# Products behind the last one that nothing reads: eight distances in memory between moving tile and weights, in two forms

## The chip, the cores and the metric

The kernel runs on one core of one Trainium2 chip. The metric is the device time of one execution in microseconds (us); of the kernel before there are two timed executions, with a median of 1193.43 us (1192.92 and 1193.94).

## The reference

Three layers are computed over 8192 tokens of 192 channels in float32: a causal mixing over seven tokens with softmaxed taps per head, a gated network, and a second network with the ELU function.

```
w   = softmax(weight)                      # 8 heads x 7 taps
x   = sum over k of w[h, k] * x[s + k - 6] # causal, per head of 24 channels
y   = (silu(x @ w_gate) * (x @ w_val)) @ w_out1      # 192 -> 1536 -> 192
out = elu(y @ w_in2) @ w_out2                        # 192 -> 2048 -> 192
```

## The kernel before, in words

Tokens are taken in 16 chunks of T = 512. Each chunk goes through a mix phase (12 steps, the gated network) and an ELU phase (8 steps j, each with two blocks of 128 hidden units). A float32 operand is kept as two float32r parts, hi and lo, and a product of two operands is made as three products: hi by hi, lo weights by hi, hi weights by lo. 192 channels are 128 and 64, so most products have 64 rows of contraction. They are issued in pairs, one on partitions 0 to 63 (TOP) and one on partitions 64 to 127 (LOW), into two banks of PSUM; `both` (L921) and `third` (L888) issue such pairs and `mm` (L885, its products are recorded at L886) issues every product.

Two forms of pair matter here. In the **up form** (`third`, also `both` in `down`), the weights are 128 columns of a weight tile and the moving tile is 512 columns of activations. In the **token form** (`by_tokens`, L948), the roles change: 128 columns of activations (`hid_hi` or `hid_lo`) are loaded as weights and the rows of `out2_w` move past them, 384 columns for the hi part and 192 for the lo part, hi and lo in turn.

The weights of the up form lie in `up1_w` and `up2_w`, their moving tiles in `in_a` and `in_b`, each with three slots of 512 columns (MAIN, CROSSED, TWICE). The sizes of all the tiles between `in_a_hi` and `hid_lo`, and of those between `up1_w_hi` and `out2_w`, are multiples of 128 columns (512 bytes), and so are the steps from one slot or weight block to the next.

Each engine runs its own instruction stream, with semaphores between them. In TensorE's stream the mix and ELU phases of chunks 2 to 14 stand in a hardware loop; what comes before and behind is written out. The last of it are `elu_phase(CHUNKS - 1)`, `elu_phase(CHUNKS)` and `last_blocks` (L977). `last_blocks` ends with products over all 128 rows into the four banks Z; each of the last four results is announced on `last_z`. Then ScalarE copies half of each bank to `result` (L660), VectorE adds the other half (L726), and SyncE and ScalarE store two blocks each (L332). SyncE at last waits until all stores have landed (L418). At the end of the program all engines meet.

At the beginning TensorE makes products on zeros and on the identity (`warm`, L1074), whose results nothing reads.

Of the kernel before, what the change touches and what calls it, by code (L numbers as in the profile page):

```python
# [28 lines left out]
P = 128  # L29


def mix_ffn_ffn(nc, x, weight, w_gate, w_val, w_out1, w_in2, w_out2, out):
    BATCH, SEQ, D = x.shape
# [4 lines left out]
    T = 512  # L38
# [34 lines left out]
    with ctx:  # L73
        def sb(name, shape, dt=F32):
            return ctx.enter_context(nc.sbuf_tensor(name, shape, dt))
# [5 lines left out]
        up1_w = {part: sb(f"up1_w_{part}", [P, PARTS, F1], F32R) for part in ("hi", "lo")}  # L81
# [5 lines left out]
        out2_w = sb("out2_w", [P, N2, 2 * D], F32R)  # L87
# [24 lines left out]
        in_a = {k: sb(f"in_a_{k}", [P, PARTS, T], F32R) for k in ("hi", "lo")}  # L112
        in_b = {k: sb(f"in_b_{k}", [P, PARTS, T], F32R) for k in ("hi", "lo")}
        MAIN, CROSSED, TWICE = range(PARTS)
# [17 lines left out]
        up = [ctx.enter_context(nc.psum_tensor(f"up{i}", [P, T], F32)) for i in range(4)]  # L132
# [3 lines left out]
        TOP, LOW = slice(0, TAIL), slice(TAIL, P)  # L136
# [747 lines left out]
        def _(pe):  # L884
            def mm(dst, lhsT, rhs, start, stop):  # L885
                return nc.tensor.matmul(dst, lhsT, rhs, start=start, stop=stop, skip_group_check=True)  # L886
# [69 lines left out]
            def down2_pair(m, k0):  # L956
                two = (k0, k0 + 1)
                turns = 2 * (N2 // 2 * m + k0 // 2)
                if k0 == 0 and is_int(m, CHUNKS - 1):
                    pe.wait_ge(result_done, summed(m))  # L960
                elif k0 == 0:
                    pe.wait_ge(y_a, 2 * (m + 2))
                    pe.wait_ge(y_b, 2 * (m + 2))
                order = ((0, 2), (1, 3), (2, 0), (3, 1))
                for turn, (b, b_low) in enumerate(order if k0 // 2 % 2 == 0 else order[::-1]):
                    if turn >= 2:
                        pe.wait_ge(z_turn, turns + turn - 1)
                    for k in two:
                        pe.wait_ge(hi2_done, N2 * m + k + 1)
                        by_tokens(k, hid_hi, b, b_low, first=k == 0)  # L970
                        pe.wait_ge(lo2_done, N2 * m + k + 1)
                        end = by_tokens(k, hid_lo, b, b_low, last=k == N2 - 1)
                    if turn < 2:
                        end.then_inc(z_turn, 1)
                end.then_inc(down2_done, 2)

            def last_blocks():  # L977
                two = (N2 - 2, N2 - 1)

                def whole(b, k, data, last=False):  # L980
                    pe.wait_ge(hi2_done, N2 * (CHUNKS - 1) + k + 1)
                    if data is hid_lo and k == N2 - 1:
                        pe.wait_ge(last_lo_done, 1)
                    elif data is hid_lo:
                        pe.wait_ge(lo2_done, N2 * (CHUNKS - 1) + k + 1)
                    w = out2_w[:, k, 0:2 * D] if data is hid_hi else out2_w[:, k, 0:D]
                    cols = slice(0, 2 * D) if data is hid_hi else slice(0, D)
                    return mm(Z[b][:, cols], data[:, k % RING, b * P:b * P + P], w, False, last)

                down2_pair(CHUNKS - 1, N2 - 4)  # L990
                for b in (0, 1):
                    whole(b, N2 - 2, hid_hi)
                    whole(b, N2 - 2, hid_lo)
                    whole(b, N2 - 1, hid_hi)
                for b in (0, 1):
                    whole(b, N2 - 1, hid_lo, True).then_inc(last_z, 1)
                for b in (2, 3):
                    for k in two:
                        whole(b, k, hid_hi)
                        last = whole(b, k, hid_lo, k == N2 - 1)  # L1000
                    last.then_inc(last_z, 1)

            def input_ready(slot, n, hi, lo, crossed):
                if slot == CROSSED:
                    pe.wait_ge(crossed, 64 * (n + 1))
                else:
                    pe.wait_ge(hi, 2 * n + 1 + (slot == TWICE))
                    pe.wait_ge(lo, 2 * n + 1 + (slot == TWICE))

            def mix_phase(n):  # L1010
# [3 lines left out]
                for f in range(2 if chunk0 else 0, N1):  # L1014
                    if chunk0 and f in UP1_AT:
                        wait_weights(pe, UP1_AT[f])

                    if chunk0 and f >= 3:
                        pe.wait_ge(mul_done, f - 1)
                    elif chunk1 or f >= 2 and not chunk0:  # L1020
                        pe.wait_ge(mul_done, N1 * n + f - 1)
                    elif not chunk0:
                        pe.wait_ge(elu_done, N2 * (n - 2) + N2 - 2 + 2 * f)
                    ready = (lambda slot: input_ready(slot, n - 1, in1_hi, in1_lo, in1_crossed)) if f == 0 \
                        else lambda slot: None
                    gate, val = project(gate_bank(f, n), val_bank(f, n), up1_w, f, input1(n), ready)
                    gate.then_inc(gate_ready, 1)
                    val.then_inc(val_ready, 1)
                    if f < 2 and is_int(n, 2) and N2 - LAG2 + 2 * f in OUT2_AT:
                        wait_weights(pe, OUT2_AT[N2 - LAG2 + 2 * f])  # L1030
                    if f < 2 and not (chunk0 or chunk1):
                        down2_pair(n - 2, N2 - LAG2 + 2 * f)
                    if f == 0 and chunk1:
                        down1(0, N1 - 2)
                        down1(0, N1 - 1)
                    if f >= LAG:
                        if chunk0 and f - LAG in OUT1_AT:
                            wait_weights(pe, OUT1_AT[f - LAG])
                        if chunk0 and f == LAG:
                            pe.wait_ge(mul_done, LAG)  # L1040
                        down1(n, f - LAG)
                    if f == N1 - 1:
                        down1(n, N1 - LAG)

            def elu_phase(n):
                last = is_int(n, CHUNKS)

                for j in range(PAIR2):
                    if is_int(n, 1) and j in UP2_AT:
                        wait_weights(pe, UP2_AT[j])  # L1050

                    if j >= 2:
                        pe.wait_ge(elu_done, N2 * (n - 1) + 2 * j - 2)
                    elif last:
                        pe.wait_ge(elu_done, N2 * (n - 1) - 2 + 2 * j)
                    else:
                        pe.wait_ge(mul_done, N1 * (n + 1) - 1 + j)
                    ready = (lambda slot: input_ready(slot, n - 1, in2_hi, in2_lo, in2_crossed)) if j == 0 \
                        else lambda slot: None
                    even, odd = project(gate_bank(j), val_bank(j), up2_w, j, input2(n - 1), ready)  # L1060
                    even.then_inc(h2_ready, 1)
                    odd.then_inc(h2_ready, 1)
                    if j == 0 and last:
                        for k in range(N2 - LAG2, N2, 2):
                            down2_pair(n - 2, k)
                    elif j == 0:
                        down1(n, N1 - 2)
                        down1(n, N1 - 1)
                    if j >= 2:
                        if is_int(n, 1) and 2 * j - LAG2 in OUT2_AT:  # L1070
                            wait_weights(pe, OUT2_AT[2 * j - LAG2])
                        down2_pair(n - 1, 2 * j - LAG2)
# [39 lines left out]
            elu_phase(CHUNKS - 1)  # L1112
            elu_phase(CHUNKS)
            last_blocks()


# [16 lines left out]
```

## Time and profile before

| what | value |
|---|---|
| median of two executions | 1193.43 us |
| the profiled execution, its own time | 1192.35 us |
| its span, first to last instruction | 1190.5 us |
| TensorE products busy | 1184.2 us, 99% of the span |
| VectorE, GpSimd, ScalarE busy | 65%, 59%, 56% |
| granted TensorE clock, mean | 1.000 |

The profiled execution took 1.85 us more than its span; that is time outside the first and last instruction. Its own time is 1.08 us below the median. A busy time is the union of the recorded spans of an engine's instructions; ends of products are modelled, so how fast TensorE works is better read from the distance between starts.

### The profile page before, as it was taken

To read this page: it belongs to the slowest core of one execution; us is meant where nothing else is said; L and a number is where in the kernel's file an instruction comes from. 1 tells how busy PE (TensorE), PEld (TensorE's weight loads), DVE (VectorE), ACT (ScalarE), POOL (GpSimd) and SP (SyncE) were. 2 spreads that over 40 slices of the span, in tenths; PEclk is the share of its full clock that TensorE was granted. 3 is DMA by queue.
4 is the path that set the end of the run, shared out by engine and by line. 5 is a ranking of instruction groups with operands and counts; after the bars stand their busy time and mean duration, and the time that the engine had idled before them with its cause. 6 is when DMAs were issued, how large, how long until landed. Compare 5 with 4: busy or idle time off the path is not lost.

```text
span 1190.5 us, 31414 instructions
## 1 busy us (share of the span) xinstructions
PE 1184.2 (99%) x11804; PEld 1021.5 (86%) x11804; DVE 777.2 (65%) x1193; ACT 664.6 (56%) x1113; POOL 704.5 (59%) x520
## 2 busy tenths in 40 slices
PE   8999999999999999999999999999999999999999
PEld 7888889898888988889888898888988889888898
DVE  7887565685656766567665766657667475675675
ACT  6557555464554646546465564655646555465565
POOL 6389566474654746557465474654756556475565
PEclk9999999999999999999999999999999999999999
DMA  8422011121111211012110021100212002120110
GB/s 179 114 50 46 12 33 35 31 44 27 25 23 31 44 31 26 18 31 44 31 35 14 26 44 31 35 18 22 44 31 44 9 22 44 31 44 9 32 33 15
DMA packets 103956, 43.38 MB, mean 36 GB/s; under 512 B 75888, under 2 KB 93936, under 8 KB 103920
## 3 DMA queue, kind: packets, MB, share of 16 engines
q1 hardware_dynamic: 103104, 42.29, 16.5%
q10 hardware_dynamic: 816, 0.59, 0.2%
q8 instruction: 24, 0.39, 0.1%
q14 instruction: 12, 0.10, 0.0%
HBM read 16.12 MB, written 6.29 MB: 19 GB/s over the span
## 4 chain that ended last, share of the span: by engine, by line
PE 99%; DVE 1%; DMA 0%; ACT 0%; issue 0%; DVEq 0%; ACTq 0%
PE up L886 55%; PE down L886 43%; DMA taps_raw<-weight_dram 0%; DVE in_a_lo L854 0%; DVE in_a_lo L859 0%; PE down L1092 0%; ACT hidden L635 0%; DVE hidden L748 0%; DVE hid_lo L729 0%; ACT in_a_hi L640 0%; DVE in_b_lo L702 0%; DVE stage L726 0%; ACT stage L660 0%; ACT taps_exp L626 0%; DVE taps_head L834 0%
## 5 line engine op out<-in xcount | busy, mean ns | idle before, releaser
L444 POOL TENSOR_TENSOR hid_lo<-hidden,hid_hi 128x512 fp32r<-128x512 f32 x435 | 607.7, 1408 | 460.0 <-ACT hid_hi L583 299.4
L886 PE MATMUL down<-out_w,hid_hi 64*128 64x384 f32 x2040 | 300.0, 355 | 0.0
L748 DVE TENSOR_TENSOR hidden<-act,up 128x512 f32<-128x512 f32 x191 | 130.9, 686 | 238.4 <-ACT act L566 238.4
L886 PE MATMUL down<-out_w,hid_lo 64*128 64x192 f32 x2040 | 256.2, 247 | 0.0
L788 DVE TENSOR_SCALAR act<-up 128x512 f32<-128x512 f32 x256 | 164.9, 686 | 105.7 <-PE up L886 103.8
L886 PE MATMUL up<-in_b_hi,up_w_hi 64*128 64x512 f32 x1128 | 222.0, 390 | 0.0
L886 PE MATMUL up<-in_b_lo,up_w_hi 64*128 64x512 f32 x1128 | 221.3, 389 | 0.0
L886 PE MATMUL up<-in_b_hi,up_w_lo 64*128 64x512 f32 x1128 | 220.6, 388 | 0.0
L583 ACT ACTIVATE hid_hi<-hidden 128x512 fp32r<-128x512 f32 x192 | 121.6, 633 | 177.2 <-DVE hidden L748 160.2
L617 ACT ACTIVATE hid_hi<-hidden 128x512 fp32r<-128x512 f32 x256 | 157.0, 629 | 97.0 <-DVE hidden L804 80.2
L602 ACT ACTIVATE act<-act 128x512 f32<-128x512 f32 x256 | 156.1, 631 | 88.0 <-DVE act L788 88.0
L886 PEld LDWEIGHTS down<-out_w,hid_lo 64*128 64x128 f32 x2040 | 195.3, 187 | 5.3
L886 PEld LDWEIGHTS down<-out_w,hid_hi 64*128 64x128 f32 x2040 | 191.8, 184 | 5.4 <-issue 0.2
L566 ACT ACTIVATE act<-up 128x512 f32<-128x512 f32 x191 | 114.2, 598 | 146.0 <-PE up L886 144.7
L804 DVE SCALAR_TENSOR_TENSOR hidden<-act,up 128x512 f32<-128x512 f32 x256 | 168.8, 681 | 36.6 <-POOL hid_lo L444 29.3
L886 PE MATMUL down<-hid_hi,out_w 64*128 64x512 f32 x1152 | 163.1, 388 | 0.0
L886 PE MATMUL up<-in_a_hi,up_w_hi 64*128 64x512 f32 x786 | 155.8, 393 | 0.8 <-ACT in_a_hi L640 0.8
L886 PE MATMUL up<-in_a_lo,up_w_hi 64*128 64x512 f32 x786 | 155.1, 391 | 0.3 <-DVE in_a_lo L859 0.3
L886 PE MATMUL up<-in_a_hi,up_w_lo 64*128 64x512 f32 x786 | 153.4, 387 | 0.0
L696 DVE SCALAR_TENSOR_TENSOR mixed<-x_t,taps,mixed 128x512 f32<-128x512 f32 x192 | 141.7, 778 | 0.0
L886 PEld LDWEIGHTS down<-hid_hi,out_w 64*128 64x128 f32 x1152 | 108.1, 184 | 23.7
L886 PEld LDWEIGHTS up<-in_b_lo,up_w_hi 64*128 64x128 f32 x1128 | 105.8, 184 | 23.3
(98 smaller groups left out, 1082.6 us busy)
## 6 DMA issues: line engine op xcount, KB each, us to landing
x_raw<-x_dram SPq DMA_DIRECT2D x136, 64.0 KB, 2.2
out_dram<-stage SPq DMA_DIRECT2D x15, 384.0 KB, 2.7
in_b_hi<-in_b_hi SPq DMA_DIRECT2D x32, 128.0 KB, 2.3
in_b_lo<-in_b_lo SPq DMA_DIRECT2D x32, 128.0 KB, 2.3
swapped<-halves SPq DMA_DIRECT2D x32, 128.0 KB, 2.3
in_a_hi<-in_a_hi SPq DMA_DIRECT2D x30, 128.0 KB, 2.3
in_a_lo<-in_a_lo SPq DMA_DIRECT2D x30, 128.0 KB, 2.3
stage<-w_out_dram SPq DMA_DIRECT2D x7, 384.0 KB, 3.9
```

Of the source, the lines that this page charges most:

```text
L444: return pool.tensor_tensor(hid_lo[:, slot, :], hidden[:, s, :], hid_hi[:, slot, :].bitcast(F32), ALU.subtract)
L566: nc.scalar.activation(act[:, f % 2, :], gate_bank(f, n)[:, :], ACT.Silu)\
L583: nc.scalar.activation(hid_hi[:, f % RING, :], hidden[:, f % 2, :], ACT.Copy)\
L602: nc.scalar.activation(act[:, k % 2, :], act[:, k % 2, :], ACT.Exp).then_inc(exp_done, 1)
L617: nc.scalar.activation(hid_hi[:, k % RING, :], hidden[:, k % 2, :], ACT.Copy)\
L696: v.scalar_tensor_tensor(mixed[:, part, :], src, tap, mixed[:, part, :], ALU.mult, ALU.add).then_inc(mix_step, 1)
L748: v.tensor_tensor(hidden[:, f % 2, :], act[:, f % 2, :], val_bank(f, n)[:, :], ALU.mult)\
L788: v.tensor_scalar(act[:, k % 2, :], elu_bank(k)[:, :], 0.0, None, ALU.min)\
L804: v.scalar_tensor_tensor(hidden[:, k % 2, :], act[:, k % 2, :], -1.0, elu_bank(k)[:, :], ALU.add, ALU.max).then_inc(elu_done, 1)
L886: return nc.tensor.matmul(dst, lhsT, rhs, start=start, stop=stop, skip_group_check=True)
```

## The change

Behind `last_blocks()` in TensorE's stream a new function `spare_time()` is called. Nothing else is changed. It makes, without a wait and without a semaphore, 128 pairs in the up form and then 64 times two token-form pairs (hi and lo).

```diff
                         last = whole(b, k, hid_lo, k == N2 - 1)
                     last.then_inc(last_z, 1)
 
+            def spare_time():
+                line = 16
+                flat = {k: in_a[k][:, :, :].rearrange("p s t -> p (s t)") for k in ("hi", "lo")}
+                upper, lower = up[1], up[2]
+                for r in range(8):
+                    for i in range(16):
+                        both(upper, lower, up1_w["hi"][:, MAIN, i % 8 * P:(i % 8 + 1) * P],
+                             flat["hi"][:, r * line:r * line + T], True, True)
+                for r in range(8):
+                    for i in range(8):
+                        for part, cols in (("hi", 2 * D), ("lo", D)):
+                            held = flat[part][:, r * line:r * line + P]
+                            for bank, rows in ((upper, TOP), (lower, LOW)):
+                                mm(bank[:, 0:cols], held[rows], out2_w[rows, i, 0:cols], True, True)
+
...
             elu_phase(CHUNKS)
             last_blocks()
+            spare_time()
```

The moving tile of the up form and the held tile of the token form start r times 16 elements (64 bytes) into `in_a`, for r from 0 to 7. The banks `up[1]` and `up[2]` and the tile `in_a` are not used by any other instruction at that time.

## Rows read from the trace of the kernel before

**Rows 1.** The page: span, busy time and instructions of TensorE, granted clock in 40 slices.

```profile
span 1190.5 us, 31414 instructions
PE 1184.2 (99%) x11804; PEld 1021.5 (86%) x11804; DVE 777.2 (65%) x1193; ACT 664.6 (56%) x1113; POOL 704.5 (59%) x520
PEclk9999999999999999999999999999999999999999
```

**Rows 2.** The page: the chain that ended last, by engine.

```profile
PE 99%; DVE 1%; DMA 0%; ACT 0%; issue 0%; DVEq 0%; ACTq 0%
```

**Rows 3.** Timeline of the end: start us, length us, engine, line, operation, tiles.

```profile
1187.18 0.36 PE L886 MATMUL down<-out_w,hid_hi 128*128 128x384 f32 x1
...
1187.38 0.25 PE L886 MATMUL down<-out_w,hid_lo 128*128 128x192 f32 x1
1187.66 0.33 ACT L660 ACTIVATE stage<-down 128x192 f32<-128x192 f32 x1 [0.24 <-PE down L886]
1187.67 1.08 ACTq L332 DMA_DIRECT2D out_dram<-stage  x2
1188.03 0.35 DVE L726 TENSOR_TENSOR stage<-stage,down 128x192 f32<-128x192 f32 x1 [0.21 <-ACT stage L660]
```

**Rows 4.** Waits of SyncE's queue, from 1150 us: total, times, longest.

```profile
SPq L418 <- DMA out_dram<-stage: 1.9, 1, 1.9
```

**Rows 5.** Timeline of TensorE, up form in the last ELU phase.

```profile
1173.98 0.41 PE L886 MATMUL up<-in_b_hi,up_w_hi 64*128 64x512 f32 x2
1174.24 0.39 PE L886 MATMUL up<-in_b_hi,up_w_lo 64*128 64x512 f32 x2
...
1175.40 0.39 PE L886 MATMUL up<-in_b_hi,up_w_hi 64*128 64x512 f32 x2
1175.62 0.39 PE L886 MATMUL up<-in_b_hi,up_w_lo 64*128 64x512 f32 x2
1175.85 0.39 PE L886 MATMUL up<-in_b_lo,up_w_hi 64*128 64x512 f32 x2
```

**Rows 6.** The same timeline, token form behind it, weight loads too at its end.

```profile
1176.08 0.34 PE L886 MATMUL down<-out_w,hid_hi 64*128 64x384 f32 x2
...
1176.26 0.25 PE L886 MATMUL down<-out_w,hid_lo 64*128 64x192 f32 x2
...
1176.35 0.36 PE L886 MATMUL down<-out_w,hid_hi 64*128 64x384 f32 x2
...
1178.07 0.36 PE L886 MATMUL down<-out_w,hid_hi 64*128 64x384 f32 x2
1178.09 0.19 PEld L886 LDWEIGHTS down<-out_w,hid_lo 64*128 64x128 f32 x2
1178.26 0.25 PE L886 MATMUL down<-out_w,hid_lo 64*128 64x192 f32 x2
1178.27 0.19 PEld L886 LDWEIGHTS up<-in_b_hi,up_w_hi 64*128 64x128 f32 x2
1178.35 0.41 PE L886 MATMUL up<-in_b_hi,up_w_hi 64*128 64x512 f32 x2
```

**Rows 7.** Stretches (start:end, length, PE and PEld busy, VectorE, ScalarE, GpSimd, granted clock).

```profile
1120.00:1187.70 67.70, 67.63 (x764) 61.55 (x760) 45.79 (x73) 40.86 (x74) 43.76 (x34) 1.00 0.08 19
```

**Rows 8.** The tile of zeros at the start: products that nothing reads, min/median/max ns.

```profile
L886 PE MATMUL up<-halos x12: 421/421/579, 1.1 to 3.6; 128*128 128x128 f32 x12
```

**Rows 9.** The page: instruction fetch over the whole span: packets, MB, share.

```profile
q8 instruction: 24, 0.39, 0.1%
```

## The prediction

> **What bounds the kernel now.** I read the page first: TensorE's products are busy for 1184.2 of 1190.5 us [rows 1], and the chain that ended last is TensorE to 99% [rows 2]. So whatever is put into TensorE's stream costs its own length, except for what fits under the tail that follows the last product. The timeline of the end shows that tail. The last product starts at 1187.38 and ends at 1187.63; a copy, an add and a store of 1.08 us of issue follow, and the last add ends at 1188.38 [rows 3]. SyncE then waits 1.9 us for the stores to land [rows 4], and the span ends at 1190.5. The tail from the end of the last product to the end of the span is 2.9 us. It holds nothing of TensorE, so that is all the cover the new work has.
>
> **What the change adds.** It removes and moves nothing. No wait is added, no semaphore is raised, no DMA is issued, and behind the new products TensorE has nothing that another engine waits for except the meeting at the end of the program. The four announcements of the last results are made before the new work, in the same order, so the copies, adds and stores begin when they began before. They run beside the new products without a price: they use the four down banks and the result tile, the new products the up banks, `in_a` and weights. Even if they took twice their 2.9 us they would be over long before TensorE.
>
> **Up form: 128 pairs.** In the last ELU phase a pair of 64 rows and 512 columns starts at 1174.24, and the eighth after it, the first product of the token form, starts at 1176.08 [rows 5, 6]: 1.84 us for eight, 0.230 us each. A pair is recorded as x2 in one row with 0.39 us of length, so the two halves run together and the next pair starts before the ends. 128 times 0.230 is 29.4 us. The bounds are two rows of the same stretch: the shortest step is 0.22 (1175.40 to 1175.62), giving 28.2 us, the longest 0.26 (1173.98 to 1174.24, right behind a token form), giving 33.3 us. I take 0.230, the mean of eight steps of the same form.
>
> **Token form: 64 times hi and lo.** From 1176.35 to 1178.35 there are seven hi-and-lo rounds: 2.00 us, 0.286 each [rows 6]. The new rounds have the same shapes (384 and 192 columns, 128 columns held, two halves) in the same order. 64 times 0.286 is 18.3 us. Within a round the hi step is 0.20 and the lo step 0.09. The first round after an up form takes only 0.27 (1176.08 to 1176.35), its hi step 0.18 where the later ones take 0.19 to 0.20. What differs is that the loads behind a lo product of 192 columns come late: the load for the up form starts at 1178.27, only 0.08 before its product at 1178.35, and lasts 0.19 [rows 6]. So the lower bound is 0.27, or 17.3 us; the upper bound is a round in which one load of 0.19 is wholly exposed, 0.48, or 30.4 us. The steady 0.286 is seven rounds of the very same form, so I take it.
>
> The Trainium skill, TensorE: Matmul & The Clock Gate, Back-to-back issue gap, gives N / 2.4 + 2.5 ns for a product at full clock, and its Part 2 says that the next weights load over a port of their own and steal nothing from the running product. By that the sum would be 128 times 216 ns and 64 times 245 ns, an estimate of 43.3 us in place of 47.7. The trace does not agree here in size: its steps are 230 and 286 ns.
>
> **The sum.** 29.4 + 18.3 = 47.7 us of starts. The first new pair can start about 0.18 us behind the last product's start, as the last lo product follows its hi product by 0.20 [rows 3]: at 1187.56. The last of the 47.7 us is a lo step of 0.09 whose product lasts 0.25 [rows 6], so the last product ends at 1187.56 + 47.7 - 0.09 + 0.25 = 1235.4. The meeting of the engines was 0.5 us at most behind the landing of the stores (the last add's end and the wait give 1188.38 + 1.9 = 1190.3 [rows 3, 4], and the span ended at 1190.5); I take 0.25. The span becomes 1235.65, 45.1 us more. On the profiled execution's own time that is 1192.35 + 45.1 = 1237.5 us; that execution lies 1.08 us below the median of 1193.43, and on the median it is **1238.5 us**, 3.8% slower.
>
> **What stays the same, and what hides it.** The granted clock is at the full level, 2.4 GHz, in all slices [rows 1] and in the last 68 us, with 67.63 of 67.70 us busy [rows 7]; the new work joins that without a gap, so I cost the clock at nothing. The written-out code grows by 512 products and as many loads. The same kind of written-out code runs from 1120 us on with the same steps and 0.07 us idle in all [rows 7], and the fetch of instructions is 24 packets in the whole span [rows 9]; the fetch goes on beside the products and I cost it at nothing. If that cover failed, each new packet would cost microseconds of standstill, and I leave that to the upper end of the range.
>
> **What the trace cannot show.** All moving tiles and all weights of the kernel lie at distances that differ by multiples of 512 bytes, since every slot and block is a multiple of 128 columns. The new work goes through eight positions within these 512 bytes, in steps of 64. So one position is shown (r = 0 is that of the products before), and seven are not. Below, they could be cheaper, by no more than the shortest rows allow. Above, a position at which the reads of moving tile and of weights get in each other's way would expose the load of 0.19 us: 0.42 a pair in place of 0.230 and 0.67 a round in place of 0.286. One such position of eight costs 16 x 0.19 + 8 x 0.38 = 6.1 us, all seven 43 us. I take no extra, as the nearest rows are the shown position's, and keep both ends.
>
> **The rivals.**
>
> *One position clashes.* A single position, or two at half of the price each, adds 6.1 us: **1244.6 us**. For it: the steps at the shown position are not all alike (0.22 to 0.26 [rows 5]), so something small depends on where the operands lie. Against it: every step, in hundreds of different blocks, is within that. Chance 0.14. All seven clash: 1281 us, chance 0.02.
>
> *Loads hide wholly.* With no load in the way at any position the up form goes at 0.22 and the token form at 0.27: 28.2 + 17.3 = 45.5 us, 2.2 less than the sum, **1236.3 us**. This is the direction of the page's rule above, by whose figures alone it would be an estimate of 1234.1. For it: a token form that follows long products has its first step shorter [rows 6]. Against it: in steady alternation the steps are 0.286 to the hundredth. Chance 0.08.
>
> *Not slower: products that nothing reads are dropped.* If the build left out products without a reader, the last instruction of TensorE would stay at 1187.6 and the time at **1193.4 us**. It would decide wherever more than half of the 47.7 us is dropped: the 2% line of 23.9 us is crossed once 26.5 us of new work remain (26.5 less 2.7 of cover). Against it: at the start of the kernel twelve products on zeros have no reader either, and all twelve stand in the trace with 421 ns [rows 8]. Chance 0.02.
>
> *The work lands in a standstill of TensorE,* by a lower clock or a late fetch. At half of the clock all of the new work would take twice as long, about 1286 us. There is nothing for it in the stretch before [rows 7]. Chance 0.02.
>
> **How the numbers follow.** The forecast's own chance is 0.72; with it go 1236.3 to 1241 us (up form at 0.25 in place of 0.230 would add 2.6). The range must hold eight in ten: it takes in the rival of hiding loads at its low end, with an offset between chips of a microsecond or two like the one between the two timed executions (1.0 us), and the single clash at its high end: 1234 to 1246 us. Left out are the larger clash, the standstill and the dropped products, with 0.06, and what I have not thought of. About 2%, 24 us, is what a measurement of this kernel can tell from no change. Only the dropped products end within it; nothing ends faster, since nothing is taken away. Slower 0.97, same 0.02, faster 0.01.
>
> **What would show it.** In the profile after, TensorE has 12316 products; the first pair on `in_a_hi` starts near 1187.6, the steps are 0.23 to near 1217, then rounds of 0.286 to near 1235, and the span ends 0.2 to 0.3 behind the last product. Each group of sixteen pairs should take 3.7 us and each group of eight rounds 2.3 us, for all eight positions; the copies, adds and stores stand at the same times as before. The prediction is wrong if a group takes clearly more or less than its neighbours, if a gap stands between last product and first new one, or if what comes before 1187 us has moved.

## The result, and the profile after

The changed kernel takes 1238.63 us (two executions, 1237.39 and 1239.87), the kernel before 1193.43. The ratio is 1.0378, 95% interval [1.0361, 1.0394]: slower by 45.2 us, where 45.1 were forecast. The profiled execution took 1237.39 us with a span of 1235.6.

The page of the kernel after, to be held against the lines of [rows 1, 2]:

```profile
span 1235.6 us, 32438 instructions
PE 1232.4 (100%) x12316; PEld 1069.4 (87%) x12316; DVE 777.1 (63%) x1193; ACT 664.7 (54%) x1113; POOL 704.5 (57%) x520
...
DVE  7787665756756566675756766575675656666620
ACT  6557465554645546465554646555464554646520
POOL 5389465565746547465564746556474654746620
...
q8 instruction: 28, 0.46, 0.2%
...
PE 99%; DVE 0%; ACT 0%; issue 0%; DVEq 0%; ACTq 0%
```

TensorE has 512 products more and 48.2 us more of busy time, while the busy times of the other engines moved by 0.1 us at most. Their last slice is empty, for there TensorE works alone. Four packets of instructions more were fetched than in [rows 9]. The clock stayed at its full level in the new work, as this stretch of it shows (start:end, length, PE busy, products, clock, DMA):

```profile
1191.40:1195.10 3.70, 3.70 (x35) 1.00 0.00 0
```

The chain of waits of the kernel after from 1180 us on (start us, us, what):

```profile
3 pieces in order of time: start us, us, what
1179.82 0.46 PE up L886 x4
1180.28 7.02 PE down L886 x80
1187.30 48.05 PE up L886 x512
```

The copies and stores that ended the chain before [rows 3] are no longer in it. The new products are one piece of 48.05 us with no gap. Its beginning, in the timeline (start us, length us; a `[` tells the idle time ahead):

```profile
1186.85 0.36 PE L886 MATMUL down<-out_w,hid_hi 128*128 128x384 f32 x1
...
1187.05 0.25 PE L886 MATMUL down<-out_w,hid_lo 128*128 128x192 f32 x1
1187.23 3.74 PEld L886 LDWEIGHTS up<-in_a_hi,up_w_hi 64*128 64x128 f32 x33 [0.16 <-issue]
1187.23 3.94 PE L886 MATMUL up<-in_a_hi,up_w_hi 64*128 64x512 f32 x31
1187.34 0.33 ACT L660 ACTIVATE stage<-down 128x192 f32<-128x192 f32 x1 [0.24 <-PE down L886]
1187.34 1.08 ACTq L332 DMA_DIRECT2D out_dram<-stage  x2
1187.70 0.35 DVE L726 TENSOR_TENSOR stage<-stage,down 128x192 f32<-128x192 f32 x1 [0.21 <-ACT stage L660]
```

Its end, TensorE alone:

```profile
1234.58 0.39 PE L886 MATMUL up<-out_w,in_a_hi 64*128 64x384 f32 x2
1234.78 0.28 PE L886 MATMUL up<-out_w,in_a_lo 64*128 64x192 f32 x2
1234.87 0.39 PE L886 MATMUL up<-out_w,in_a_hi 64*128 64x384 f32 x2
1235.06 0.28 PE L886 MATMUL up<-out_w,in_a_lo 64*128 64x192 f32 x2
```

The first new pair starts 0.18 us behind the last old product, and the copy, the stores and the add have the same lengths and order as in [rows 3]. The last round is 0.29 us (1234.58 to 1234.87), as in [rows 6]. The last product ends at 1235.34 and the span 0.25 us later.

From the start stamps of the products the two forms can be timed group by group. This table is worked out from the trace after; a group is the sixteen pairs or eight rounds of one r:

```
r                        0      1      2      3      4      5      6      7     sum
up form, ns a pair     236.2  232.9  232.9  229.4  230.1  232.3  233.0  227.9   29.68 us
token form, ns a round 284.0  286.9  284.1  284.1  286.5  286.9  284.1  284.6   18.25 us
```

Together they are 47.9 us; the prediction had 29.4 + 18.3 = 47.7. The 236.2 of r = 0 is not the rate of that position: the very first pair, behind a product over 128 rows, takes 336 ns to the next start, and the other fifteen take 229.6 on the mean.

### The profile page after: what moved, and what is told of

It is laid out like the page before. It is cut to its first block, busy times and chain, and to the rows that moved or that the text cites. A ratio compares the mean times of both kernels' runs of the same rounds, so it can differ in the third digit from the quotient of the medians.

```text
span 1235.6 us, 32438 instructions
## 1 busy us (share of the span) xinstructions
PE 1232.4 (100%) x12316; PEld 1069.4 (87%) x12316; DVE 777.1 (63%) x1193; ACT 664.7 (54%) x1113; POOL 704.5 (57%) x520
## 4 chain that ended last, share of the span: by engine, by line
PE 99%; DVE 0%; ACT 0%; issue 0%; DVEq 0%; ACTq 0%
PE up L886 57%; PE down L886 42%; DVE in_a_lo L854 0%; DVE in_a_lo L859 0%; PE down L1107 0%; ACT hidden L635 0%; DVE hidden L748 0%; DVE hid_lo L729 0%; ACT in_a_hi L640 0%; DVE in_b_lo L702 0%; DVE halos L811 0%; DVE halos L864 0%; DVEq L713 0%; ACTq L631 0%
## 5 line engine op out<-in xcount | busy, mean ns | idle before, releaser
L886 PE MATMUL up<-in_a_hi,up_w_hi 64*128 64x512 f32 x1042 | 185.8, 392 | 0.8 <-ACT in_a_hi L640 0.8
```

## The experiments

Where an interval stands, the time is a median, and the interval is the 95% interval of the ratio to the kernel before, timed on the same chip. A time without an interval is one execution.

**1. The up form alone**

```diff
-                for r in range(8):
-                    for i in range(8):
-                        for part, cols in (("hi", 2 * D), ("lo", D)):
-...
```

> Only the 128 pairs in the up form, the token form left out. Length theory (every product behind the last one costs its step of the start-to-start distance, less 2.6 us that fit under the stores): 29.7 - 2.6 = 27.1 us over the kernel before, about 1220.5 us. Rival, that the tail of 2.9 us is not cover but is pushed behind the new work: 29.7 us more, 1223.1. Rival, that the token form takes more than its starts show (its 18.2 us include time that the up form caused): the two parts alone do not add up to the whole plus 2.6 us.

Measured: 1220.13 us, ratio 1.0227 [1.0211, 1.0243], 27.0 us over the 1193.15 of the kernel before. The rival of 29.7 us would be a ratio of 1.0249, outside the interval. The groups took what they took in the change to within 0.2 ns a pair. The chain of waits of this run:

```profile
1187.42 29.80 PE up L886 x256
```

**2. The token form alone**

```diff
-                for r in range(8):
-                    for i in range(16):
-                        both(upper, lower, up1_w["hi"][:, MAIN, i % 8 * P:(i % 8 + 1) * P],
...
```

> Only the 64 rounds in the token form, the up form left out. Length theory: 18.2 - 2.6 = 15.6 us over the kernel before, about 1209.0 us, and rounds of 0.284 to 0.287 us. Rival, tail pushed behind: 18.2 more, 1211.6. If the order of the positions does not matter, the groups of eight rounds take what they took behind the up form: 2.27 to 2.30 us.

Measured: 1209.26 us, ratio 1.0134 [1.0118, 1.0149], 16.1 us more. The rival of 18.2 us (1.0153) is outside. The first group took 296 ns a round, all of it from its first round with 369, and the other seven 284.1 to 286.9, as in the change. The two parts give 27.0 + 16.1 = 43.1 us; each has the cover of 2.6 us taken off, the whole has it once, so 43.1 + 2.6 = 45.7 stand against the 45.2 measured. The 0.5 us between them is less than the intervals of either (about 2 us each way), so no effect of one part on the other is shown.

**3. Ten pairs only**

```diff
-                for r in range(8):
-                    for i in range(16):
+                for r in range(1):
+                    for i in range(10):
```

The token form is left out.

> Only 10 pairs in the up form, all at r = 0. Length theory: the last of them ends at 1187.56 + 10 x 0.232 + 0.16 = 1190.0 us on the scale of the trace before, ahead of the landing of the stores at about 1190.1; so the time does not move (0 to 0.2 us). Rival, that new work behind the last product costs its length from the first product on: 2.3 us more, a ratio of 1.0019.

Measured: 1193.28 us, ratio 0.9999 [0.9990, 1.0008]. The 1.0019 of the rival is outside. The timeline of this run and SyncE's last wait:

```profile
1188.91 0.25 PE L886 MATMUL down<-out_w,hid_lo 128*128 128x192 f32 x1
1189.09 2.17 PEld L886 LDWEIGHTS up<-in_a_hi,up_w_hi 64*128 64x128 f32 x20 [0.16 <-issue]
1189.09 2.60 PE L886 MATMUL up<-in_a_hi,up_w_hi 64*128 64x512 f32 x20
1189.20 0.33 ACT L660 ACTIVATE stage<-down 128x192 f32<-128x192 f32 x1 [0.24 <-PE down L886]
...
```
```profile
SPq L418 <- DMA out_dram<-stage: 1.8, 1, 1.8
```

2.60 us of new work lie beside copy, add and stores; TensorE is done at 1191.7, and the span ends at 1192.1 with the stores, 2.9 us behind the end of the last old product at 1189.16. So the cover is real: here 2.5 us, from 1189.16 to 1191.69, cost nothing, close to the 2.6 us that the sum gave it.

**4. The same work ahead of the last products**

```diff
                 down2_pair(CHUNKS - 1, N2 - 4)
+                pe.wait_ge(elu_done, N2 * CHUNKS)
+                spare_time()
...
             last_blocks()
-            spare_time()
```

> The same products stand ahead of the last twelve of the kernel (between the last pair of token-form steps of last_blocks and the products over 128 rows) behind a wait for the last ELU results, which should long be there. Length theory: the cover of the tail is lost, so the whole 47.9 us of the new starts are paid, 1193.4 + 47.9 = 1241.3, and 0 to 0.3 us more for the wait; 2.6 us over the change. Rival, that position in the stream does not matter because the stores' tail was never cover: the same as the change, 1238.6. On the halves of a pair: in the kernel before both start within 4 ns, in the change the second lags by up to 63 ns. If the 128-row products ahead of them cause this, the lag is gone here; if the new products themselves do (same columns for both halves, start and stop on each), it is there again.

Measured: 1242.19 us, ratio 1.0412 [1.0395, 1.0430], 48.75 us more; 1.0401 was expected. The change's own ratio, from another session, was 1.0378 [1.0361, 1.0394]; the two intervals just fail to meet. The trace accounts for 47.81 of the 48.75 us, the length of the new work; that the rest lies in what wanders from run to run is likely, and not shown. The chain of waits has the new work and the tail one behind the other:

```profile
1184.89 47.81 PE up L886 x512
1232.70 2.47 PE down L886 x16
1235.17 0.02 issue
1235.20 0.34 ACT stage L660
1235.54 0.02 issue
1235.56 0.35 DVE stage L726
```

Experiments 3 and 4 show the cover from both sides: work that fits under the tail is free, and the work of the change, moved in front of it, is paid in full. The first pair took 255 ns to the next start, behind a product over 64 rows, where it took 336 in the change behind one over 128 rows. On the halves of a pair, the second started 3 to 4 ns behind the first throughout, as in the kernel before.

**5. Both products of a pair on the same rows**

```diff
-                        both(upper, lower, up1_w["hi"][:, MAIN, i % 8 * P:(i % 8 + 1) * P],
-                             flat["hi"][:, r * line:r * line + T], True, True)
+                        for bank in (upper, lower):
+                            mm(bank[:, :], up1_w["hi"][TOP, MAIN, i % 8 * P:(i % 8 + 1) * P],
+                               flat["hi"][TOP, r * line:r * line + T], True, True)
...
-                            for bank, rows in ((upper, TOP), (lower, LOW)):
+                            for bank, rows in ((upper, TOP), (lower, TOP)):
```

> As the change, but the second product of each pair also stands on partitions 0 to 63, so both halves of a pair go through the same rows of the array (it computes the same product twice, into two banks). Theory that a pair costs one step because its halves run beside each other: now each product takes a step of its own, 0.215 to 0.230 us in the up form and about 0.14 on the mean in the token form: 2 x 47.9 = 95 us of starts and 1193.4 + 95 - 2.6 = 1286 us. Rival, that the pairs' starts are only recorded together and the products queue up anyway: 1238.6 us as before.

Measured: 1286.23 us in one execution, 1286 expected. The chain of waits has the work at twice its length, and the timeline shows a round of 0.57 us in place of 0.29:

```profile
1188.45 95.81 PE up L886 x512
```
```profile
1282.95 0.53 PE L886 MATMUL up<-out_w,in_a_hi 64*128 64x384 f32 x2
1283.33 0.36 PE L886 MATMUL up<-out_w,in_a_lo 64*128 64x192 f32 x2
1283.53 0.53 PE L886 MATMUL up<-out_w,in_a_hi 64*128 64x384 f32 x2
```

The number of products did not change, only the rows that they use. The step of the prediction, one step for a pair rather than for a product, is what this shows.

**6. Adding up instead of starting anew**

```diff
-                             flat["hi"][:, r * line:r * line + T], True, True)
+                             flat["hi"][:, r * line:r * line + T], r == 0 and i == 0, r == 7 and i == 15)
```

and the same for the token form.

> As the change, but the new products add up in their banks: start is set on the first pair of each form alone and stop on the last alone. Length theory: nothing changes, 1237 to 1240 us, 227 to 236 ns a pair. Rival, that the start flag costs (the first pair of a group with start took 0.26 us in the kernel before): steps go down to 0.225 and the lag between the halves vanishes, up to 1.5 us less.

Measured: 1237.07 us in one execution. All sixteen groups took what they took in the change, to the tenth of a nanosecond a pair. The flags cost nothing, and the lag between halves is the same as well, so it does not come from them.

**7. The eight positions in reverse order**

```diff
-                for r in range(8):
+                for r in reversed(range(8)):
```

in both forms.

> The eight positions in the reverse order, r from 7 to 0, in both forms; everything else as in the change. Theory that the small differences between groups (3.65 to 3.78 us for sixteen pairs, 2.27 to 2.295 for eight rounds) belong to the position: the groups' times come in the reverse order, the slow ones (236 and 233 ns a pair) now last. Theory that they belong to the time since the start (stores under way, the halves of a pair settling): the first groups are again the slow ones. The whole is the same within 0.5 us in both, 1237 to 1239 us.

Measured: 1238.32 us in one execution. In the order run, with r named:

```
r                        7      6      5      4      3      2      1      0
up form, ns a pair     235.2  233.4  232.1  229.7  228.3  233.3  232.1  229.7
token form, ns a round 281.4  284.8  286.8  286.6  284.5  284.4  287.0  285.7
```

The whole of the first group's excess is its first pair, whichever position it has: that pair takes 337 ns here and 336 in the change, and the fifteen behind it take 228.4 at r = 7 here and 229.6 at r = 0 there. So the steps go by position from the second pair on, and the positions repeat every four, that is every 256 bytes: about 230, 232, 233, 228 ns for r modulo 4 = 0, 1, 2, 3. The token form goes by position too: about 286.5, 287, 284 and 284.5.

**8. Steps of four bytes**

```diff
-                line = 16
+                line = 1
```

> As the change, with steps of 1 element (4 bytes) in place of 16 (64 bytes) between the eight positions, so that seven of eight tiles start within a 64-byte line. Length theory: no difference, 1237 to 1240 us and 227 to 236 ns a pair. Rival, that a moving tile which does not start on a 64-byte line needs one more read for each line or clashes with the weight reads: the seven shifted groups of sixteen pairs take 3.9 us and more in place of 3.7, and the first does not.

Measured: 1240.47 us in one execution, 0.5 above what was expected. What it has more than the profiled execution of the change (3.1 us) lies ahead of the new work for the most part: its last old product starts at 1189.81, in the change at 1187.05. The new up form took 29.86 us against 29.68, the token form 18.30 against 18.25. No group comes near 3.9 us, so the rival is out. But the step is not blind to these bytes. Worked out from the start stamps:

```
bytes from r = 0         0      4      8     12     16     20     24     28
up form, ns a pair     236.2  236.1  235.2  228.2  231.2  234.5  233.1  231.5
```

The first number has the slow first pair in it again (229.6 without). Four bytes cost 6.5 ns a pair and twelve bytes give back 1.4, as much as any step of 64 bytes. The eight positions of the change are thus a sample and not the whole pattern. No control was run for these distances.

**9. The weights move, the activations stay**

```diff
+                w_flat = up1_w["hi"][:, :, :].rearrange("p s f -> p (s f)")
...
-                        both(upper, lower, up1_w["hi"][:, MAIN, i % 8 * P:(i % 8 + 1) * P],
-                             flat["hi"][:, r * line:r * line + T], True, True)
+                        at = r * line + i % 8 * P
+                        both(upper, lower, w_flat[:, at:at + P], flat["hi"][:, 0:T], True, True)
```

In the token form the held tile stays at r = 0 and the moving rows of `out2_w` start r times 16 elements later.

> As the change, but the activation tile stays at r = 0 and the weight tile moves by r times 64 bytes instead (moving tile and weights in the up form, held tile and moving weights in the token form change their part). Distance theory: the groups take in the order of r = 0, -1, -2, -3 of the change, so 230, 228, 233, 232 ns a pair and again. Address theory, moving tile alone: all eight groups of the up form take the same, 230. Whole time the same in both within 1 us, 1237 to 1240.

Measured: 1239.84 us in one execution. The up form took, in ns a pair from r = 0 on: 236.7, 227.3, 233.2, 231.8, 229.3, 227.4, 233.2, 231.9. The first has the slow first pair in it again. The others are 227, 233, 232, 229 and again, the order of r = -1, -2, -3, 0. In the up form the distance between moving tile and weights counts, and not the place of the moving tile.

The token form took 282.8, 290.1, 286.5, 286.5, 286.0, 290.1, 286.5, 286.6 ns a round. By distance, r = -1, -2, -3 should have given about 284.5, 284 and 287. So the theory does not hold for the token form as it does for the up form; what counts there is open.

**10 to 12. The distance in the kernel itself**

The new products are left out in all three. 48 or 32 unused columns are laid ahead of the activation tiles, or 48 ahead of all tiles:

```diff
+        pad = sb("pad", [P, 48])
         in_a = {k: sb(f"in_a_{k}", [P, PARTS, T], F32R) for k in ("hi", "lo")}
```
```diff
+        pad = sb("pad", [P, 48])
         up1_w = {part: sb(f"up1_w_{part}", [P, PARTS, F1], F32R) for part in ("hi", "lo")}
```

> The kernel before, without the new products, with 48 unused columns (192 bytes) laid ahead of in_a_hi, so that every activation tile (in_a, in_b, hid_hi, hid_lo and what is between and behind) lies where r = 3 lay against the weights. Position theory (the step of an up-form pair goes with the place of the moving tile within 256 bytes against the weights: 230 at r = 0, 232, 233, 228 at r = 3, measured in the new products): 3840 pairs in the kernel take about 2 ns less each, 7.7 us, and the token form 0 to 2 us less: 1184 to 1186 us, ratio 0.993. Rival, that it is a property of those particular blocks and not of the place: no difference, 1193.4.

> The same with 32 unused columns (128 bytes), the place of r = 2. Position theory: 3840 pairs take about 3 ns more each, 11.5 us, the token form up to 2 us less: 1203 to 1205 us, ratio 1.009. Rival: no difference, 1193.4.

> The kernel before with the 48 unused columns laid ahead of all tiles, so that weights and activations move together: their distances stay, their own addresses change by 192 bytes. If the distance between moving tile and weights sets the step, nothing changes: 1193.4, mean step of an up-form pair 230.1 ns. If the address of the moving tile alone sets it, this goes as the variant with the activation tiles moved alone: 1184 to 1186.

Measured, with the mean steps between 60 and 1180 us worked out from the start stamps:

| kernel | us | ratio to before | up form, ns a pair | token form, ns a round |
|---|---|---|---|---|
| before | 1193.51 | 1 | 230.15 | 283.8 |
| 48 columns ahead of the activations | 1182.69 | 0.9908 [0.9891, 0.9924] | 227.92 | 281.5 |
| 32 columns ahead of the activations | 1206.99 | 1.0111 [1.0095, 1.0128] | 234.16 | 281.9 |
| 48 columns ahead of all tiles | 1192.94 | 0.9996 [0.9986, 1.0005] | 230.14 | 283.9 |

The direction was as expected in all three: faster, slower, unchanged. Both shifts of the activations gave more than expected, 1182.69 against 1184 to 1186 and 1206.99 against 1203 to 1205. The means of the up form include the first pair behind each token form, which takes 252 to 256 ns; without it they are 229.2, 227.1, 233.4 and 229.2.

The stretch from 50 to 1100 us, TensorE alone (length, busy, products, clock), of the kernel before, then with 48, then with 32 columns ahead of the activations:

```profile
50.00:1100.00 1050.00, 1050.00 (x10504) 1.00 0.15 32
```
```profile
50.00:1100.00 1050.00, 1050.00 (x10592) 1.00 0.15 32
```
```profile
50.00:1100.00 1050.00, 1050.00 (x10400) 1.00 0.15 32
```

TensorE is busy for all of the 1050 us in each, at the same clock and with the same traffic of DMA. It only gets through 88 products more, or 104 fewer, in the same time. So a busy share of 100% hides the whole effect, and the count of products in a fixed stretch shows it. The sums agree: 3840 pairs times -2.23 ns and 1024 rounds times -2.3 ns are -10.9 us (measured -10.8), and 3840 times +4.0 with 1024 times -1.9 are +13.4 us (measured +13.5). The version with 48 unused columns ahead of the activations beats both kernels, by 0.9% the one before.

The Trainium skill (TensorE: Matmul & The Clock Gate, Part 2, Step-by-step) says that the next weights are read over a port of their own and take nothing from the running product. The measurements do not bear that out as it stands: how far apart the two lie, modulo 256 bytes, moved the step of the up form from 227.9 to 234.2 ns, so reading the one is not without effect on the other. Whether the load takes time from the product, or something else does, no run here shows.

## Why the prediction was right, point by point

**The bound.** TensorE's stream sets the end, so work behind its last product costs its length less the tail. Experiments 1, 2 and 5 show the first (27.0, 16.1 and 92.8 us for 29.7, 18.2 and 95.7 of starts), experiments 3 and 4 the second.

**The cover.** The sum used 2.6 of the 2.9 us. Adding ten pairs changed the time by 0.1 us, in an interval of -1.2 to +1.0 us.

**The first start.** The prediction put it 0.18 us behind the last old start, and it was 0.18. The row given for it, a lo product 0.20 behind its hi product, is not the right one, since a product of 192 columns is otherwise followed after 0.09 [rows 6]. The kernel before has the same change between 64 and 128 rows, the other way, with the same 0.16 us in which no weights are loaded:

```profile
1184.92 0.25 PE L886 MATMUL down<-out_w,hid_lo 64*128 64x192 f32 x2
1185.10 0.19 PEld L886 LDWEIGHTS down<-out_w,hid_hi 128*128 128x128 f32 x1 [0.16 <-issue]
1185.10 0.44 PE L886 MATMUL down<-out_w,hid_hi 128*128 128x384 f32 x1
1185.38 0.25 PE L886 MATMUL down<-out_w,hid_lo 128*128 128x192 f32 x1
```

The agreement is luck. These rows also show what the sum left out: the first step behind such a change is 0.28 and not 0.20, and in the new work it was 0.336 and not 0.230.

**The up form.** Taken at 0.230 us a pair from eight steps, it came to 0.2319, 29.68 for 29.4 us. Of the difference 0.11 us is the first pair, and the rest the mean over positions (228 to 233).

**The token form.** Taken at 0.286 us, it came to 0.285, 18.25 for 18.3 us. Steady rounds were the right row to take, and not the first round with 0.27. (The upper bound should read 64 x 0.476 = 30.5 us, not 30.4.)

**Concurrency of a pair.** Experiment 5 shows it: on the same rows the same number of products takes twice the time.

**What was costed at nothing.** Copies, add and stores kept their lengths, the fetch of instructions took four packets more without a gap, and the clock stayed at its full level; its mean was 0.999 or 1.000 in every run. What a packet that is not covered would cost, no run shows; those of q8 took 0.9 to 1.4 us each in the trace before.

**The positions that the trace could not show.** The prediction took no extra, bounded them with a wholly exposed weight load (6.1 us for one position, 43 for seven), and gave the clash 0.14. That bound was some fifty times too wide: the worst of the eight places costs 3 ns a pair more than the one shown (4 in the padded kernel), not 190. Its remark that the steps "are not all alike, so something small depends on where the operands lie" came true, but not by its evidence: the 0.26 is the first pair behind a token form, which takes 252 to 256 ns at each of the three distances that were tried in the whole kernel. Over eight positions the small effects nearly cancel, which is why the sum does not show them.

**The rival of hiding loads.** It did not happen: no position reached 0.22 and 0.27.

**The rival of dropped products.** All 512 stand in the trace. The prediction's condition for it was loose: by its own figures the 2% line is crossed once 21.2 of the 47.7 us are dropped, which is less than half.

**Where the agreement is luck.** The part of the kernel ahead of the new work wanders from run to run: the last old product started at 1187.38 before, 1187.05 in the change, 1186.8 to 1189.8 in the others. Half a microsecond or more of the fit of 1238.63 to 1238.5 is therefore chance. The 47.9 us of the new work is what the argument can claim.

## What to carry to other kernels

Where TensorE is busy from end to end, cost new products by start-to-start steps of the same shapes in steady alternation, counted in concurrent pairs, and take off only what fits between its last product and the end. A busy share of 100% says nothing about how long a step is: count products in a fixed stretch. If moving tiles and weights are all multiples of 512 bytes apart, try 64, 128 and 192 bytes of unused columns between the two groups of tiles: the one distance that all share is one draw of several, and of the two others tried here in the whole kernel one was faster and one slower. A form of product other than the up form may go by something else.

## What the runs showed of the hardware that was not expected

- The distance between moving tile and weights, modulo 256 bytes in steps of 64, moves the step of a 64 x 512 pair: about 230, 232, 233 and 228 ns at 0, 64, 128 and 192 bytes more than this kernel's own. Its sign was shown by moving the weights, its independence of absolute places by moving all tiles. Steps of four bytes moved it as much (228 to 236 ns, one run, experiment 8). Why it is so was not tried.
- The first pair behind a product over 128 rows starts 0.18 us after it and takes 336 ns to the next start (337 in reverse order); behind a token form over 64 rows it starts 0.08 us after it and takes 252 to 256. This is the whole of the slow first group.
- The 192 bytes gave more in the kernel than expected (10.8 us for 7.4 to 9.4), and the 128 bytes cost more (13.5 for about 10). There the mean step was 234.2 ns, 4.0 more than before, where 3 had been taken.
- The halves of a pair are not tied to each other. In the kernel before they start 3.3 ns apart. In the change the second falls behind in the first group and then stays 36 to 64 ns late for good (up to 81 in experiment 8); the rows of its end above show it as 0.39 and 0.28 us of length in place of the 0.36 and 0.25 of [rows 6]. It costs nothing by itself: from r = 4 on the groups take the same with the lag (the change) and without it (experiment 4). It appeared when r = 0 came right behind the products over 128 rows, not when r = 7 did (experiment 7), not for the token form (experiment 2), and not ahead of those products (experiment 4). What starts it is open.
